# Column halves for the w_out product, column quarters for the second expert product, the combine and the stores, and fewer unused products in the drain

## The chip, the cores and the metric

The kernel runs on one core of a Trainium2 chip. The metric is the device time of one execution in microseconds (us), median of three runs. TensorE (PE), VectorE (DVE), ScalarE (ACT) and the DMA queues work side by side and are tied by semaphores. All data are fp32.

## The reference, cut to what matters

Three layers follow each other. First a chunked attention with eight memory keys (4 batches, 8 heads, 768 positions, 64 wide). Then a dense layer with a rational activation, then a soft mixture of 8 experts with 4 slots each:

```python
# x: 3072 x 512, the attention's output
h = x @ w_in                                   # 3072 x 2048
g = (a0 + a1*h + a2*h*h + a3*h*h*h) / (1 + abs(b0)*abs(h) + abs(b1)*h*h + 1e-6)
y = g @ w_out                                  # 3072 x 512
logits = y @ phi                               # 3072 x 32
d = softmax(logits, axis=0)                    # over all tokens
slot_input = (d.T @ y).reshape(8, 4, 512)
for e in range(8):
    slot_out[e] = maximum(slot_input[e] @ w1[e], 0) @ w2[e]      # 512 -> 1024 -> 512
c = softmax(logits, axis=1)                    # over the 32 slots
out = c @ slot_out                             # 3072 x 512
```

The softmax over all tokens means that no expert can start before the last token is through. w1 and w2 hold 16.8 MB each, and the output 6.3 MB.

## The kernel before, in words

**The stream of tiles.** The 3072 tokens are 24 tiles of 128 (`N`). For each tile TensorE makes the attention's scores and products, transposes, the hidden layer in four parts of 512 columns (`hidden`, lines 413 to 429, three products for each block: w_hi and w_lo, x_hi and x_lo), transposes of g (`g_transposes`, L355 by its helper), the logits by the folded weights w_out phi (`logits`, L449), and `slots` (L472), the running sum of d.T g. `step` (lines 492 to 564) interleaves the work of tiles n to n + 2. x_hi and x_lo each have two places, for even and odd tiles.

**The drain.** After the last tile, `step(B, 0)` and `step(B, 1)` finish what is left of tiles 22 and 23. Between the products that wait for other engines stand unused ones on constants (`spin_drain`, L361), four, three and one in a place.

**The slot stage.** The accumulator is transposed, copied (L888), multiplied by w_out over all 512 columns (L599, 16 products, four blocks f of four), scaled and copied to `sip` (L893), turned by four products (L605) and copied to `siT` (L895).

**The experts.** Expert weights stream through a ring of 11 stages (lines 106 to 130) of 2 MB, each of two pairs of halves; a half is 0.5 MB. Places are cut from memory that earlier phases leave: w_hi and w_lo, the attention's inputs, x, hs, g and wout. All loads and stores are issued by SyncE (lines 258 to 346), in order, each behind a wait for what frees its place. Stages 0 to 7 hold w1, 8 to 15 w2. `expert_hidden` (L615) makes the hidden slots of two groups of four experts, one expert in each 32-column strip of TensorE's array (128*32); `expert_turns` transposes them.

**Second product, combine, stores.** `expert_out` (L652) multiplies by w2. Its stages are ordered by column half `ch` of the 512 output columns, group and half of the hidden rows: stages 8 to 11 give columns 0 to 255, 12 to 15 the rest, in products 256 columns wide. VectorE adds the two groups under masks (L1140, L1143), `slot_rows` (L661) spreads the 32 rows, ScalarE copies them to `s_rows` (L912), and `combine` (L681) multiplies by the transposed c: a 32-row strip for each of four token tiles (32*128). A copy out of PSUM takes one bank, two token tiles of 256 columns. VectorE and ScalarE take turns (L1148, L916), 12 copies for each half, over banks that come round after 5 or 7. There are nine stores: three of 1 MB for the first half, six of 0.5 MB for the second. The order on TensorE is written out at lines 686 to 709:

```python
            expert_out(13, (0, 1))
            slot_rows(0)
            expert_out(13, (2, 3))
            combine(0, 0)
            expert_out(14)
            combine(0, 1)
            expert_out(15, (0, 1))
            combine(0, 2)
            expert_out(15, (2, 3))
            slot_rows(1)
            for a in range(PAIRS // 4):
                combine(1, a)
```

Of the kernel before, what the change touches and what calls it, by code (L numbers as in the profile page):

```python
# [5 lines left out]
def build(nc, qT_d, kw_d, vw_d, w_in, w_out, w_outT, cst_d, w1, w2, out):  # L6
    f32 = mybir.dt.float32
# [10 lines left out]
    N = B * T  # L18
# [11 lines left out]
    with ExitStack() as ctx:  # L30
# [23 lines left out]
        x_hi = sb("x_hi", [P, 2, KD * P], f32r)  # L54
        x_lo = sb("x_lo", [P, 2, KD * P], f32r)
# [18 lines left out]

        xn = sc
# [28 lines left out]
        assert offset["x_hi"] >= in_att + ATT * QB and offset["hs"] >= in_att + (ATT + LATE) * QB  # L104
# [5 lines left out]
        pairs += [in_att + QB * ATT, in_g, in_tmp, in_wout, in_wout + 2 * QB, (in_tmp + 2 * QB, in_wout + 7 * QB)]  # L110
# [17 lines left out]
        def landings(stage):  # L128
# [3 lines left out]
        HC = DM // 2  # L132
        PAIRS = N // 2
        o_place = [nc.alloc_sbuf_tensor_at("o_a", [P, 8, 2 * HC], f32, offset=in_wout),
                   nc.alloc_sbuf_tensor_at("o_b", [P, 4, 2 * HC], f32, offset=in_tmp + QB),
                   nc.alloc_sbuf_tensor_at("o_c", [P, 12, 2 * HC], f32, offset=in_early)]

        def o_out(ch, j):
            if ch:
                return o_place[2][:, j, :]  # L140
            return o_place[0][:, j, :] if j < 8 else o_place[1][:, j - 8, :]
# [14 lines left out]
        o_bank = [at[:, 0, :], at[:, 1, :], gb[:, :], at[:, 2, :], sl[:, :], hb[:, 0, :], hb[:, 1, :]]  # L156
        o_banks = (5, 7)
        h_banks = [hb[:, 0:2, :], at[:, 0:2, :]]
        y_bank = [[at[:, 2, :], sl[:, :]], [hb[:, 0, :], hb[:, 1, :]]]
# [94 lines left out]

        block = ctx.enter_context(nc.Block())
# [3 lines left out]
        def _(sp):  # L259
            def load_pair(stage, x, part=None):  # L260

                i = stage - 8
                src = w1[2 * (stage // 4) + x, stage % 4] if i < 0 else w2[i // 4, 2 * (i // 2 % 2) + x, i % 2]
# [33 lines left out]
            for n in range(2, N):  # L297
                load_qk(n)
                load_v(n)
                if n < 2 + EARLY // 2:  # L300
                    load_pair((n - 2) // 2, n % 2)
                elif n == 2 + EARLY // 2:
                    sp.dma_start(place(3, 0), w1[0, 3][:, 0:QUARTER]).then_inc(stage_ready[3], 16)
# [7 lines left out]
            sp.dma_start(place(3, 1), w1[0, 3][:, QUARTER:2 * QUARTER]).then_inc(stage_ready[3], 16)  # L311
# [7 lines left out]
            load_pair(8, 0)  # L319
# [4 lines left out]
            sp.wait_ge(si_psum, 1)  # L324
            load_pair(9, 1)
            sp.wait_ge(si_psum, 2)
            load_pair(10, 0)
            sp.wait_ge(si_psum, 4)
# [10 lines left out]
            STORES = ((0, 0, 4), (0, 4, 4), (0, 8, 4)) + tuple((1, 2 * k, 2) for k in range(6))  # L339
            for ch, j, count in STORES:  # L340
                sp.wait_ge(o_dve, PAIRS // 2 * ch + (j + count) // 2)
                sp.wait_ge(o_act, PAIRS // 2 * ch + (j + count) // 2)
                where = o_place[2] if ch else o_place[j // 8]
                k = j if ch else j % 8
                sp.dma_start(out[ch, :, j:j + count, :], where[:, k:k + count, :]).then_inc(stored, 16)
            sp.wait_ge(stored, 16 * len(STORES))
# [3 lines left out]
        def _(pe):  # L350
# [116 lines left out]
            def slots(b, t):  # L467
                n = b * T + t
                pe.wait_ge(dk_sb, n + 1)
                need(pe, acc_done, n)  # L470
                for f in range(FC):
                    i = mm(sl[NS * f:NS * f + NS, :], dk[:, :], g[:, t % 3, 512 * f:512 * f + 512],  # L472
# [19 lines left out]
            def step(b, t):  # L492
# [104 lines left out]
            for f in range(FC):  # L597
                for j in range(4):
                    i = mm(sl[NS * j:NS * j + NS, :], aT[:, j, NS * f:NS * f + NS], wout[:, 4 * f + j, :],  # L599
                           start=f == 0, stop=f == FC - 1)  # L600
                i.then_inc(si_psum, 1)
            spin_drain(B, 2, 3)
            pe.wait_ge(si_sb, 1)
            for kd in range(KD):
                i = mm(mb[:, NS * kd:NS * kd + NS], sip[:, kd * P:kd * P + P], srep[:, 0:NS], start=True, stop=True)  # L605
            i.then_inc(siT_psum, 1)
            spin_drain(B, 2, 1)
# [32 lines left out]
            def expert_out(stage, js=range(4)):  # L640
                ch, grp, fth = (stage - 8) // 4, (stage - 8) // 2 % 2, stage % 2
                cs = slice(HC * ch, HC * ch + HC)
                if js[0] == 0:
                    pe.wait_ge(stage_ready[stage], 32 if stage == 15 else 16 * landings(stage))
                for j in js:
                    ft = 4 * fth + j
                    if ch == 0 and j == 0:
                        pe.wait_ge((hT_act, hT_dve)[fth], grp + 1)
                    if stage == 15 and j == 2:
                        pe.wait_ge(last_ready, 32)  # L650
                    for c in range(4):
                        i = mm(y_bank[ch][grp][NS * c:NS * c + NS, 0:HC], hT[grp][:, ft, NS * c:NS * c + NS],  # L652
                               place(stage, c // 2 * 2 + j // 2)[:, HC * (2 * (c % 2) + j % 2):][:, 0:HC], start=ft == 0, stop=ft == FET - 1)
                if js[-1] == 3:
                    i.then_inc(stage_used, 1)

            def slot_rows(ch):
                cs = slice(HC * ch, HC * ch + HC)
                pe.wait_ge(y_sb, 2 * ch + 2)
                pe.wait_ge(hT_dve, 2)  # L660
                mm(mb[:, cs], srep[:, :], so[:, cs], start=True, stop=True).then_inc(rep_psum, 1)  # L661

            def combine(ch, a):
                cs = slice(HC * ch, HC * ch + HC)
                if a == 0:
                    pe.wait_ge(s_kept, ch + 1)
                if ch == 0 and a == 0:
# [3 lines left out]
                nb = o_banks[ch]  # L671
                for m in range(2):
                    for r in range(4):
                        j = 4 * a + r
                        q = PAIRS * ch + (j - nb if j >= nb else -1)
                        if m == 0 and q >= 0:
                            pe.wait_ge((o_dve, o_act)[q % 2], q // 2 + 1)
                        if m == 0 and q >= 1:
                            pe.wait_ge((o_act, o_dve)[q % 2], (q + 1) // 2)
                        rows = slice(NS * r, NS * r + NS)  # L680
                        i = mm(o_bank[j % nb][:, HC * m:HC * m + HC], cT[rows, 2 * a + m, :], s_rows[rows, cs],  # L681
# [524 lines left out]
```

## Time and profile before

| | us |
|---|---|
| median of three runs | 519.40 (519.39 to 519.45) |
| the profiled execution | 519.27 |
| its span on the core | 517.5 |
| TensorE busy | 503.0 |
| VectorE busy | 441.0 |
| ScalarE busy | 399.0 |

The span is what the profile covers; the profiled execution's own time is 1.8 us longer. In the page's second part the span is cut into 40 slices of 12.9 us, and a digit gives the busy share in tenths. A matmul of fp32 data stands as two records, and a row's `x` counts records. In a row of the timeline, the first number is the start in us, the second is the time from the first start to the last end, and `[0.34 <-DVE dk L994]` says that the engine had been idle and for what. `128*32` is the strip of the array that a product uses.

### The profile page before, as it was taken

What the parts mean: (1) busy time and instruction counts of PE and PEld (TensorE: products, weight loads), DVE (VectorE), ACT (ScalarE), POOL (GpSimd) and SP (SyncE); (2) the same over time, 40 slices, a digit from 0 to 9 for tenths busy, and PEclk for the clock granted to TensorE, in tenths of its full rate; (3) what the DMA queues carried; (4) which work ended last, traced back from release to release, by engine and by line L of the source; (5) the groups of instructions that cost most, each with busy time, mean ns of one, the idle gap of its engine ahead of it and who ended that gap; (6) DMA issues with size and microseconds to landing.
All of it is one profiled execution on the core that took longest, in us unless ns stands there. A gap on an engine that the chain in (4) does not pass through costs nothing.

```text
span 517.5 us, 15763 instructions
## 1 busy us (share of the span) xinstructions
PE 503.0 (97%) x6568; PEld 380.1 (73%) x6568; DVE 441.0 (85%) x821; ACT 399.0 (77%) x776; POOL 0.2 (0%) x4
## 2 busy tenths in 40 slices
PE   8899999999999999999999999999999999999993
PEld 7667777877787787778778777877877787654552
DVE  4898999999999999999999999999999999951133
ACT  2877989888888988888898888889888988921122
POOL 0000000000000000000000000000000000000000
PEclk9999999999999999999999999999999999999997
DMA  8982275366313122311313232131322214999998
GB/s 343 418 355 98 90 267 196 95 243 229 119 64 105 42 91 75 97 51 63 104 44 93 72 80 68 63 104 44 100 66 72 75 43 141 424 420 408 417 365 348
DMA packets 18934, 85.29 MB, mean 165 GB/s; under 512 B 2096, under 2 KB 2224, under 8 KB 13488
## 3 DMA queue, kind: packets, MB, share of 16 engines
q1 hardware_dynamic: 18720, 84.09, 44.2%
q8 instruction: 52, 0.85, 0.7%
q10 hardware_dynamic: 144, 0.20, 0.1%
q14 instruction: 18, 0.15, 0.1%
HBM read 77.99 MB, written 6.29 MB: 163 GB/s over the span
## 4 chain that ended last, share of the span: by engine, by line
PE 92%; ACT 2%; DMA 2%; DVE 1%; issue 1%; SPq 0%; DVEq 0%; ACTq 0%
PE hb L425 17%; PE hb L427 17%; PE hb L426 17%; PE gb L355 10%; PE sl L472 4%; PE at L355 4%; PE mb L449 4%; PE at L402 4%; PE at L378 3%; DMA g<-w_in 2%; PE at L615 1%; PE hb L615 1%; PE hb L652 1%; PE mb L457 1%; PE mb L355 1%; PE hb L361 1%
## 5 line engine op out<-in xcount | busy, mean ns | idle before, releaser
L425 PE MATMUL hb<-w_hi,x_hi 128*128 128x512 f32 x384 | 160.2, 417 | 0.8 <-DVE x_lo L955 0.8
L427 PE MATMUL hb<-w_hi,x_lo 128*128 128x512 f32 x384 | 151.7, 395 | 0.0
L426 PE MATMUL hb<-w_lo,x_hi 128*128 128x512 f32 x384 | 151.4, 394 | 0.0
L742 ACT ACTIVATE hs<-hb 128x512 f32<-128x512 f32 x96 | 57.2, 596 | 44.3 <-PE hb L427 44.3
L427 PEld LDWEIGHTS hb<-w_hi,x_lo 128*128 128x128 f32 x384 | 72.1, 188 | 17.7
L425 PEld LDWEIGHTS hb<-w_hi,x_hi 128*128 128x128 f32 x384 | 72.2, 188 | 15.0 <-issue 2.0
L426 PEld LDWEIGHTS hb<-w_lo,x_hi 128*128 128x128 f32 x384 | 72.4, 189 | 12.9
L964 DVE SCALAR_TENSOR_TENSOR h<-h,few,ab 128x512 f32<-128x512 f32 x96 | 71.9, 749 | 10.2 <-ACT h L746 9.9
L751 ACT ACTIVATE h<-h,few 128x512 f32<-128x512 f32 x96 | 70.1, 730 | 9.1 <-DVE h L964 9.1
L969 DVE SCALAR_TENSOR_TENSOR tt<-tt,cst,hs 128x512 f32<-128x512 f32 x96 | 72.2, 752 | 3.4
L979 DVE SCALAR_TENSOR_TENSOR g<-tt,cst,h 128x512 f32<-128x512 f32 x96 | 71.4, 746 | 2.3 <-ACT h L755 0.2
L744 ACT ACTIVATE ab<-hb,cst 128x512 f32<-128x512 f32 x96 | 65.8, 686 | 0.6 <-DVE h L964 0.6
L967 DVE TENSOR_TENSOR tt<-tt,hs 128x512 f32<-128x512 f32 x96 | 65.8, 685 | 0.0
L755 ACT ACTIVATE h<-h 128x512 f32<-128x512 f32 x96 | 60.7, 632 | 3.1
L355 PE MATMUL gb<-cst,g 128*128 128x128 f32 x380 | 59.7, 280 | 0.4 <-ACT gT L761 0.4
L746 ACT ACTIVATE h<-hb 128x512 f32<-128x512 f32 x96 | 57.9, 603 | 0.0
L761 ACT ACTIVATE gT<-gb 128x512 f32<-128x512 f32 x93 | 56.2, 604 | 0.7 <-PE gb L355 0.7
L962 DVE TENSOR_SCALAR tt<-hs,cst 128x512 f32<-128x512 f32 x96 | 52.1, 543 | 2.9 <-ACT hs L742 0.4
L355 PEld LDWEIGHTS gb<-cst,g 128*128 128x128 f32 x380 | 42.7, 140 | 10.4 <-issue 2.2
L355 PE MATMUL at<-cst,sc 128*128 128x128 f32 x192 | 29.7, 277 | 1.5 <-ACT sc L721 1.1
L449 PEld LDWEIGHTS mb<-gT,Wp 128*32 128x32 f32 x736 | 20.9, 110 | 13.5 <-issue 13.5
L355 PEld LDWEIGHTS at<-cst,sc 128*128 128x128 f32 x192 | 23.7, 150 | 6.1 <-ACT sc L721 1.8
(154 smaller groups left out, 540.4 us busy)
## 6 DMA issues: line engine op xcount, KB each, us to landing
place<-w SPq DMA_DIRECT2D x27, 1024.0 KB, 9.6
v_in<-v_windows SPq DMA_DIRECT2D x24, 520.0 KB, 3.7
kw<-k_windows SPq DMA_DIRECT2D x24, 512.0 KB, 4.6
qT<-q_t SPq DMA_DIRECT2D x24, 256.0 KB, 2.8
place<-w SPq DMA_DIRECT2D x10, 512.0 KB, 16.6
wout<-w_out_t SPq DMA_DIRECT2D x4, 1024.0 KB, 14.6
wout<-w_out SPq DMA_DIRECT2D x4, 1024.0 KB, 9.0
g<-w_in SPq DMA_DIRECT2D x3, 1024.0 KB, 10.3
```

The source lines that it names most:

```text
L355: return mm(dst, src, ident[0:rows, 0:rows], start=True, stop=True, is_transpose=True)
L425: mm(o, x_hi[:, p, xs], w_hi[:, f, kd, :], start=kd == 0, stop=False)
L426: mm(o, x_hi[:, p, xs], w_lo[:, f, kd, :], start=False, stop=False)
L427: i = mm(o, x_lo[:, p, xs], w_hi[:, f, kd, :], start=False, stop=kd == KD - 1)
L744: A(ab[:, :], hb[:, e, :], ACT.Abs, scale=bc[:, 0:1])
L746: A(h2[:, e, :], hb[:, e, :], ACT.Square).then_inc(h_read, 1)
L751: A(h2[:, e, :], h2[:, e, :], ACT.Ln, bias=cq[:, 0:1]).then_inc(ln_done, 1)
L755: A(h2[:, e, :], h2[:, e, :], ACT.Exp, scale=-1.0).then_inc(r_done, 1)
L964: V.scalar_tensor_tensor(out=h2[:, e, :], in0=h2[:, e, :], scalar=bm[:, 1:2], in1=ab[:, :], op0=ALU.mult, op1=ALU.add).then_inc(q_done, 1)
L967: V.tensor_tensor(tt[:, e, :], tt[:, e, :], hs[:, e, :], ALU.mult).then_inc(poly_step, 1)
L969: V.scalar_tensor_tensor(out=tt[:, e, :], in0=tt[:, e, :], scalar=pc[:, 1:2], in1=hs[:, e, :], op0=ALU.add, op1=ALU.mult).then_inc(poly_st ...
L979: V.scalar_tensor_tensor(out=g[:, t % 3, 512 * f:512 * f + 512], in0=tt[:, e, :], scalar=pc[:, 0:1], in1=h2[:, e, :], op0=ALU.add, op1=ALU ...
```

## The change: what it does

1. **x.** x_hi and x_lo become one tensor in which a tile's two halves lie together, so the place of even tiles is one half of the ring. The first half of stage 8 is issued as soon as tile 22's hidden parts are done, ahead of stages 4 to 7. The other half of that pair keeps its place behind stage 7.
2. **The drain.** Unused products 4 -> 1 and 3 -> 2 before and after the last transposes of g. The slots product of the last tile writes another PSUM bank and doesn't wait for the accumulation before it; the accumulation of tile 22 moves behind VectorE's copy of dk for tile 23.
3. **The slot stage.** The w_out product runs over columns 0 to 255, then 256 to 511, into two banks. The turn of the first half stands inside the second half, the turn of the second half behind the first stage of the expert's hidden product, and the unused products of this stage (3 and 1) go. The loads that follow si_psum wait for its new counts.
4. **Second product.** w2 is laid out on the host by column quarters (128 columns): a stage holds all 1024 hidden rows of one quarter and one group. Order of (quarter, group): (0,0) (1,0) (0,1) (1,1) (2,0) (2,1) (3,0) (3,1). A stage is 32 products of 128 columns, not 16 of 256. Both groups of a quarter share one PSUM bank.
5. **Combine, copies, stores.** For each quarter there is a set of 16 products filling four banks (four token tiles each) and one of 8 filling half of four banks. Banks come round after 5. A store follows each set: 1 MB and 0.5 MB, eight in all. The host's rearranging of the output follows.

```diff
+            def load_half(stage, half):
+                sp.dma_start(place(stage, half), (w1[half // 2, stage] if stage < 4 else w2_of(stage, half // 2))
+                             [:, QUARTER * (half % 2):QUARTER * (half % 2) + QUARTER]).then_inc(stage_ready[stage], 16)
...
+            sp.wait_ge(h_psum, (N - 1) * FC)
+            load_half(8, 0)
             for f in range(FC):
...
-            load_pair(8, 0)
+            load_half(8, 1)
...
-            sp.wait_ge(si_psum, 1)
+            sp.wait_ge(si_psum, 2)
             load_pair(9, 1)
...
+            for quarter in range(4):
+                for part in range(2):
+                    cs = slice(16 * HC * part, 16 * HC + 8 * HC * part)
+                    sp.wait_ge(o_dve, 4 * quarter + 2 * part + 2)
+                    sp.wait_ge(o_act, 4 * quarter + 2 * part + 2)
+                    sp.dma_start(out[quarter, :, cs], o_place[quarter][:, cs]).then_inc(stored, 16)
...
                 if drain:
-                    spin_drain(b, t, 4)
+                    spin_drain(b, t, 1)
                     g_transposes(*prev, 3)
-                    spin_drain(b, t, 3)
+                    spin_drain(b, t, 2)
                     logits(*prev)
...
+            def slot_turns(half):
+                pe.wait_ge(si_sb, half + 1)
+                for kd in (2 * half, 2 * half + 1):
+                    i = mm(mb[:, NS * kd:NS * kd + NS], sip[:, kd * P:kd * P + P], srep[:, 0:NS], start=True, stop=True)
+                i.then_inc(siT_psum, 1)
+            for half in range(2):
+                cs = slice(DM // 2 * half, DM // 2 * half + DM // 2)
+                for f in range(FC):
+                    for j in range(4):
+                        i = mm((sl, gb)[half][NS * j:NS * j + NS, cs], aT[:, j, NS * f:NS * f + NS], wout[:, 4 * f + j, cs],
+                               start=f == 0, stop=f == FC - 1)
+                    if half or f == FC - 1:
+                        i.then_inc(si_psum, 1)
+                    if half and f == 1:
+                        slot_turns(0)
...
+                    for j in range(4):
+                        ft = 4 * half + j
+                        for c in range(4):
+                            u = mm(y_bank[quarter % 2][NS * c:NS * c + NS, HC * grp:HC * grp + HC], hT[grp][:, ft, NS * c:NS * c + NS],
+                                   place(stage, c // 2 * 2 + half)[:, HC * (4 * (c % 2) + j):HC * (4 * (c % 2) + j) + HC],
+                                   start=ft == 0, stop=ft == FET - 1)
...
+                k = 0
+                for a in SETS[part]:
+                    for m in range(2):
+                        for r in range(4):
+                            u = o_use(quarter, part, r) - len(o_banks)
+                            if k == 0 and u >= 0:
+                                pe.wait_ge((o_dve, o_act)[u % 2], u // 2 + 1)
...
+                            i = mm(o_bank(quarter, part, r)[:, HC * k:HC * k + HC], cT[rows, 2 * a + m, :], s_rows[rows, cs],
+                                   start=True, stop=True)
...
+            expert_out(3, (0,))
+            slot_rows(0)
+            expert_out(3, (1,))
+            combine(0, 0)
+            slot_rows(1)
+            expert_out(4, (0,))
+            combine(0, 1)
+            expert_out(4, (1,))
+            combine(1, 0)
+            expert_out(5, (0,))
+            combine(1, 1)
+            expert_out(5, (1,))
+            expert_out(6, (0,))
+            slot_rows(2)
+            expert_out(6, (1,))
+            combine(2, 0)
+            expert_out(7, (0,))
+            combine(2, 1)
+            expert_out(7, (1,))
+            slot_rows(3)
+            combine(3, 0)
+            combine(3, 1)
...
+                if n == N + 1:
+                    accumulate(*tile(-3))
+                if prev2 and n not in (N - 1, N):
                     accumulate(*prev2)
...
+            def slot_sum(quarter):
+                cs = slice(HC * quarter, HC * quarter + HC)
+                dve.wait_ge(stage_used, 9 + W2_STAGES.index((quarter, 1)))
+                V.tensor_scalar(so[:, cs], y_bank[quarter % 2][:, 0:HC], emask[:, 0:1], None, ALU.mult).then_inc(y_sb, 1)
...
```

## Rows read from the trace of the kernel before

**Rows 1.** The page, second part: clock and DMA in 40 slices.
```profile
PEclk9999999999999999999999999999999999999997
DMA  8982275366313122311313232131322214999998
```

**Rows 2.** The chain of waits, from 503: start us, us, what.
```profile
503.87 0.40 DVE g L1140
...
506.08 0.55 PE at L681 x2
...
507.24 0.70 DVE o_c L1148
...
510.92 0.60 DVEq L30
```

**Rows 3.** Windows: PE, PEld, DVE, ACT, POOL busy, PEclk, DMA share, GB/s.
```profile
434.00:438.00 4.00, 4.00 (x19) 3.21 (x18) 3.64 (x7) 3.57 (x8) 0.00 (x0) 1.00 0.15 25
498.00:499.00 1.00, 1.00 (x24) 0.57 (x20) 0.84 (x2) 0.68 (x2) 0.00 (x0) 1.00 0.50 201
504.00:505.00 1.00, 0.09 (x1) 0.09 (x1) 0.75 (x2) 0.00 (x0) 0.00 (x0) 1.00 1.03 418
514.00:517.50 3.50, 0.00 (x0) 0.00 (x0) 0.00 (x0) 0.00 (x0) 0.00 (x0) 0.50 0.75 298
```

**Rows 4.** The timeline of the drain, all engines.
```profile
451.09 1.41 DVE L979 SCALAR_TENSOR_TENSOR g<-tt,cst,h 128x512 f32<-128x512 f32 x2
451.61 1.57 ACT L761 ACTIVATE gT<-at 128x512 f32<-128x512 f32 x3
...
452.38 1.06 PE L361 MATMUL hb<-cst 128*128 128x128 f32 x8
...
453.28 0.60 PE L355 MATMUL gb<-cst,g 128*128 128x128 f32 x4
...
458.06 0.33 PE L355 MATMUL hb<-cst 128*128 128x128 f32 x1
...
458.71 0.18 DVE L994 COPY dk<-hb 128x32 f32<-128x32 f32 x1
...
458.95 1.07 PE L472 MATMUL sl<-g,dk 128*32 128x512 f32 x8 [0.34 <-DVE dk L994]
```

**Rows 5.** The timeline of the slot stage, TensorE.
```profile
462.23 3.64 PE L599 MATMUL sl<-wout,gT 128*32 128x512 f32 x32
...
466.68 1.08 PE L605 MATMUL mb<-cst,g 128*128 128x32 f32 x8
...
468.12 7.07 PE L615 MATMUL hb<-place,g 128*32 128x512 f32 x64
```

**Rows 6.** The timeline of the second product and the combine, TensorE.
```profile
483.99 1.91 PE L652 MATMUL at<-place,g 128*32 128x256 f32 x32
...
492.06 2.77 PE L652 MATMUL hb<-place,g 128*32 128x256 f32 x48
494.76 0.70 PE L661 MATMUL mb<-g,cst 128*128 128x256 f32 x2
495.39 1.07 PE L652 MATMUL hb<-place,g 128*32 128x256 f32 x16
496.39 0.48 PE L681 MATMUL at<-s_rows,cT 32*128 32x256 f32 x2
...
497.46 1.93 PE L652 MATMUL hb<-place,gT 128*32 128x256 f32 x32
```

**Rows 7.** The chain of waits, one tile's logits.
```profile
432.19 0.88 PE mb L449 x32
```

**Rows 8.** Groups by form, 440 to 512 us, weight loads of the combine.
```profile
L681 PEld LDWEIGHTS at<-s_rows,cT 32*128 32x128 f32 x56 | 4.6, 183 | 2.5 <-ACT s_rows L912 0.9 <-DVE o_c L1148 0.6 <-ACT o_a L916 0.4
```

**Rows 9.** The timeline of SyncE's queue: issues.
```profile
463.36 0.33 SPq L266 DMA_DIRECT2D place<-w  x1
...
507.99 5.41 SPq L345 DMA_DIRECT2D out_dram<-o_c x6
```

More of the change, by code:

```diff
@@ L337, in _ @@
                     load_pair(15, x, part_of)
[L339 to L346, printed above, removed]
+            for quarter in range(4):
[4 more added lines that the diff above has]
+                    sp.dma_start(out[quarter, :, cs], o_place[quarter][:, cs]).then_inc(stored, 16)
+            sp.wait_ge(stored, 16 * 8)
         @block.tensor
@@ L469, in slots @@
                 pe.wait_ge(dk_sb, n + 1)
-                need(pe, acc_done, n)
+                if not (isinstance(n, int) and n == N - 1):
+                    need(pe, acc_done, n)
                 for f in range(FC):
-                    i = mm(sl[NS * f:NS * f + NS, :], dk[:, :], g[:, t % 3, 512 * f:512 * f + 512],
+                    i = mm(s_bank(n)[NS * f:NS * f + NS, :], dk[:, :], g[:, t % 3, 512 * f:512 * f + 512],
                            start=True, stop=True)
@@ L638, in combine_turns @@
                 i.then_inc(cT_psum, 1)
[L640 to L649, printed above, removed]
-                        pe.wait_ge(last_ready, 32)
[L651 to L660, printed above, removed]
-                mm(mb[:, cs], srep[:, :], so[:, cs], start=True, stop=True).then_inc(rep_psum, 1)
[L663 to L667, printed above, removed]
+            def expert_out(i, halves=(0, 1)):
+                quarter, grp = W2_STAGES[i]
+                stage = 8 + i
+                for half in halves:
+                    if half == 0:
+                        pe.wait_ge(stage_ready[stage], 32 if stage == 15 else 16 * landings(stage))
+                    elif stage == 15:
+                        pe.wait_ge(last_ready, 32)
+                    if quarter == 0:
+                        pe.wait_ge((hT_act, hT_dve)[half], grp + 1)
+                    for j in range(4):
[4 more added lines that the diff above has]
+                                   start=ft == 0, stop=ft == FET - 1)
+                if half == 1:
+                    u.then_inc(stage_used, 1)
@@ new lines, in slot_rows, with combine @@
+            def slot_rows(quarter):
+                cs = slice(HC * quarter, HC * quarter + HC)
+                pe.wait_ge(y_sb, 2 * quarter + 2)
+                if quarter == 0:
+                    pe.wait_ge(hT_dve, 2)
+                    pe.wait_ge(cT_dve, 1)
+                mm(mb[:, cs], srep[:, :], so[:, cs], start=True, stop=True).then_inc(rep_psum, 1)
+            def combine(quarter, part):
+                cs = slice(HC * quarter, HC * quarter + HC)
+                if part == 0:
+                    pe.wait_ge(s_kept, quarter + 1)
+                if quarter == 0 and part == 0:
@@ L670, in combine @@
                     pe.wait_ge(cT_dve, 1)
[L671 to L681, printed above, removed]
-                               start=True, stop=True)
-                        if m == 1:
-                            i.then_inc(o_psums, 1)
-            for kd in range(KD):
-                expert_hidden(0, kd)
+                k = 0
[5 more added lines that the diff above has]
+                                pe.wait_ge((o_dve, o_act)[u % 2], u // 2 + 1)
+                            rows = slice(NS * r, NS * r + NS)
+                            i = mm(o_bank(quarter, part, r)[:, HC * k:HC * k + HC], cT[rows, 2 * a + m, :], s_rows[rows, cs],
+                                   start=True, stop=True)
+                            if k == 2 * len(SETS[part]) - 1:
+                                i.then_inc(o_psums, 1)
+                        k += 1
+            expert_hidden(0, 0)
+            slot_turns(1)
+            expert_hidden(0, 1)
+            pe.wait_ge(siT_sb, 2)
+            expert_hidden(0, 2)
+            expert_hidden(0, 3)
             expert_hidden(1, 0)
```

157 lines of the change are left out of this document (82 added, 75 removed).

## The prediction
> **What bounds the kernel now.** I read the page first, then the busy time by stretches, then the chain of waits of the end, then the instructions in order of time. On the page the reader is to see TensorE busy in nearly every slice at the full granted clock, and the DMA line going to 9 over the last sixth [rows 1]. So there are two candidates behind about 440 us. In the chain of waits the loads do not appear: TensorE works through the second expert product with its data landed, and the last load is done when the DMA share falls to one half at 498 to 499 us [rows 3], while the last product ends at 503.87 us. What follows is a serial tail [rows 2]: slot rows on VectorE, a spread product, a copy on ScalarE, the combine from 506.08, the first copy out of PSUM at 507.24, the first of six stores at 507.99 [rows 9], the last copy at 510.92, and then only data moving: 3.15 MB left to store after 507.99. The share of 0.75 over the last 3.5 us, next to about 1.03 at full load [rows 3], puts the last byte at 514 + 3.5 x 0.75/1.03 = 516.6 us, 0.9 before the end of the span. At the 418 GB/s of a full stretch [rows 3] 3.15 MB take 7.5 us, so the data began 1.1 us behind the first issue. The tail from the last product to the end is 13.6 us, of which 7.5 is half of the output going out in one stretch. It is the tail's stores and TensorE's path to them that count; the steady state up to 450 us is not touched.
>
> **The drain (450 to 461 us).** Four unused products go. Each is two records, 0.11 us a record: 8 records stand from 452.38 to 453.28 [rows 4], so 0.22 to 0.225 each. The fourth part's transposes stood behind four of them. Their input, g of the last part, is ready at 451.09 + 1.41 = 452.50 [rows 4]; with one product they start at 452.60 and not at 453.28: 0.68 us. ScalarE's copy of them and the logits follow at the same distance, since ScalarE is done with the three earlier copies by about 453.2. The other product removed lay in that copy's shadow. Second, VectorE's copy of dk for the last tile at 458.71 stood behind an accumulation, while its transpose had ended at 458.39; the slots product started at 458.95 after 0.34 us of idling [rows 4]. Now the copy goes first, the product writes another bank and waits for no accumulation, and it starts 0.3 us sooner. The accumulation moved behind it, about 0.7 us like the 512-column copy [rows 2], lies beside a slots product of 1.07 and is hidden; if it weren't, at most 0.7 returns. Together 1.0 us. Bounds: 0.3 (the copies are the gate after all) and 1.0, and I take 1.0, because the rows name each gate.
>
> **The w_out product in halves (462 to 468 us).** Before, the product starts at 462.23, then come three unused products, the turn of sip (8 records from 466.68), one more unused product, and the first expert product at 468.12 [rows 5]: 5.89 us. The halves stream the same columns: 64 records of 256 columns take 3.46 us in another place (48 of them 492.06 to 494.76) [rows 6], as 32 of 512 do here, so 3.64 stays. ScalarE's copy of the first half (0.52 for 512 columns [rows 4]) lies beside 0.91 us of the second half's products. What is left on the path is half of the turn, 4 records, 0.52 us, and two changes of the array's shape. I price those from the same rows: 16 records of the second product take 1.00 us where 16 x 0.0541 = 0.87 would do [rows 6], so 0.13 a change. 3.64 + 0.52 + 0.26 = 4.4 us: 1.5 gained. The second half of the turn comes back behind the first hidden stage at 0.52 + 0.26 = 0.8. Net 0.7. TensorE then comes to the second expert product 1.7 us sooner, 482.3 instead of 483.99.
>
> **Loads.** Half of one stage is now asked for when tile 22 has left its x place, into a stretch where DMA is 0.15 busy [rows 3]: 0.5 MB, 1.25 us, off the saturated stretch. One load that waited for the first quarter of the w_out product is issued at about 463.6 instead of 463.36 [rows 9], since a row block is only free after its second half; the queue has work until about 464.3 by then, and data follow an issue by about a microsecond, so at most 0.5 us of the gain is lost. Before, the last load was done at about 498.5; now it is at 497 to 497.5. Its user comes behind 502, so loads stay hidden; what they cost if TensorE gained 5 us more is another matter.
>
> **The second product, combine and stores by quarters.** Product: 512 records of 128 columns. The form exists: 32 records of the logits take 0.88 us [rows 7], 0.0275 each, so 14.1 us in all, where 256 columns gave 0.0541 x 256 = 13.9. Combine: before, 16 records from 496.39 to 497.46 [rows 6], 1.07 us, of which 0.85 is streaming (0.0535 a record, as in the product) and 0.2 the change. With 128 columns no row shows it. Lower bound: 0.0275 a record, half the streaming, the logits' own interval. Upper bound: 0.0535, nothing saved, because the loaded weights stay 128 columns wide at 0.18 us a load [rows 8] and are twice as many. I take 0.0275: the load overlaps between the four row groups already (four loads of 0.183 pass in 4 x 0.0535 = 0.21), and 128-wide loads with 128 columns pass at 0.11 in the unused products [rows 4]; four groups side by side make 0.0275. Slot rows: the before form took 0.63 (494.76 to 495.39) [rows 6] for 256 columns; with half 0.42, and there are three before the last product's end instead of one.
>
> Path from the start of the second product to its end, after: products 14.1, nine pieces followed by another shape x 0.13 = 1.2, the turn of the hidden part 1.0 as before, slot rows 3 x 0.42 = 1.3, combine 144 records x 0.0275 = 4.0 and 6 x 0.2 = 1.2, and two waits of 0.25 where a combine's second set needs the bank whose copy is VectorE's second (two copies of 0.65 against a 1.0 us half stage). Sum 23.2 us; before it was 503.87 - 483.99 = 19.9. The last product ends at 482.3 + 23.2 = 505.5, which is 1.6 us later than now.
>
> **Tail after.** From the last product to the combine now 2.21 us [rows 2]; with 128 columns each of the four steps shortens, estimated 1.7. Combine of the first set: 32 records 0.9 and 0.3 of latency; two VectorE copies 0.7 + 0.6; store issued at 505.5 + 1.7 + 1.15 + 1.3 = 509.7. The second set waits for those copies, 0.5 and 0.8 us, issued at 511.0, while the first set's data still move. Data: 509.7 + 1.1, then 1.57 MB in 3.8 us: 514.6. With 0.9 the span ends at 515.5. Earlier quarters don't hold it up: 497.3 + 4.7 MB in 11.4 us is 508.7, before 510.8. The span shortens by 2.0 to 2.1 us; the profiled execution took 519.27, 1.77 of it around the span of 517.5, so 517.2. The median of the runs, 519.40, is 0.13 above the profiled one, less than I can resolve.
>
> **Rivals.** (1) *The combine becomes bound by weight loads.* Each combine product keeps 128 stationary columns, and there are 96 instead of 48. If 0.0535 a record stands, 144 x 0.026 = 3.7 us are added before the last product's end and 0.8 + 0.2 behind it: 517.2 + 4.7 = 521.9, slower. It decides from about 0.039 a record, where the gain is gone. For: the load row is 0.183 us, longer than half the streaming. Against: four pass in 0.21 already. The Trainium skill, page "TensorE: Matmul & The Clock Gate", section "Part 2: What happens when you issue a matmul", says that loading weights costs by the number of columns and not by rows, so a 32-row load costs as much as a full one; by its 107 ns per 128 columns and with nothing in parallel the combine alone would take 192 x 0.107 = 20.5 us, an estimate from that page. The trace disagrees with the serial form, since 16 records take 1.07 with everything [rows 6], where that form would need 1.7. Chance 0.12.
> (2) *The removed unused products hid real waits*: TensorE then idles where it spun, the 0.7 us of the drain and 0.3 of the w_out stage don't come: 518.2. For: ScalarE's three copies (to 453.18) end close to the new start. Chance 0.15.
> (3) *Changes of shape overlap with following loads*, or the eviction waits vanish: 1 to 1.5 us less, 515.9. The limit is the data: 497 + 15.1 for all stores + 0.9 = 513, or 514.8 as a time. Chance 0.12.
> (4) *The clock.* It was granted at the full 2.4 GHz throughout, through the idle 0.9 us at 504 too [rows 3], and stands at one half (1.2 GHz) only in the last stretch, with no product left [rows 3]. With eight unused products fewer, a fall in the drain would double some 4 us of work: 521. Chance 0.03.
> (5) *The diff does nothing*: the tail is moved, not shortened, 519.2. Chance 0.05.
>
> **Numbers.** Forecast 0.53 for 517.2, own range 516.4 to 518.2. 0.2% is 1.04 us and about what can be told from no change, so faster means under 518.4: forecast, (3) and most of (2): 0.77. Same: a piece of (2) and (5), 0.08. Slower: (1), (4): 0.15. Range 515.4 to 519.4: it takes in (2), (3) and (5), and leaves out (1) and (4).
>
> **What would show it.** The transposes of the last part at 452.6 (not 453.3); the first expert product at about 465.6 and the second at 482.3; the combine's 16 records in 0.65 us, 32 in 1.1 (at 0.0535: 1.05 and 1.9); the last product's end at 505.5; stores of the last quarter issued at 509.7 and 511.0; a DMA pause before 510.8. The prediction is wrong if the last product ends beyond 507.5, if loads stop TensorE in stages 14 or 15, or if DMA is busy without pause from 440 us to the end, in which case data and not TensorE set the end.

## The result and the profile after

The changed kernel takes 522.33 us (521.92 to 522.70), the kernel before 519.39 (519.30 to 519.45) beside it: a ratio of 1.0055 (1.0043 to 1.0067). It is slower by 2.9 us where 2.2 us less were forecast. The profiled execution took 522.7 us, its span 520.9.

The page, second and third part:
```profile
PE   8899999999999999999999999999999999899884
PEclk9999999999999999999999999999999999999999
DMA  8992275367223122312322131322223117999996
q8 instruction: 55, 0.90, 0.7%
```
TensorE's line of the kernel before:
```profile
PE   8899999999999999999999999999999999999993
```
Against [rows 1] the DMA line has the same shape, and the clock is full in the last slice too. TensorE's line has 8s where the kernel before had 9s: in the slice of the drain (442.8 to 455.8 us), whose unused products are gone, and in the two from 481.8 to 507.9, where the second product and the combine are. The page doesn't say why. Queue 8 carries instructions: 55 packets of 16 KB, 52 in the kernel before.

The chain of waits says it (start us, us, what):
```profile
490.81 2.06 issue
...
497.92 1.33 issue
...
503.94 0.95 issue
...
511.21 0.36 DVE g L1201
...
512.00 0.50 PE mb L691 x2
...
512.86 0.37 PE hb L709
...
514.06 1.28 DVE o L1210 x2
...
516.35 0.33 DVEq L30
```
The lower part answers to [rows 2]: sum, spread, combine and copies, in the forecast's order and close to its length. The upper three lines are new. "issue" is time in which the engine waited for nothing that the profile shows. The timeline of TensorE shows where they lie:
```profile
452.70 0.60 PE L375 MATMUL gb<-cst,g 128*128 128x128 f32 x4
...
458.09 1.06 PE L493 MATMUL at<-g,dk 128*32 128x512 f32 x8
...
461.37 1.93 PE L628 MATMUL sl<-wout,gT 128*32 128x256 f32 x32
...
464.10 0.63 PE L621 MATMUL mb<-cst,g 128*128 128x32 f32 x4
...
482.08 1.93 PE L679 MATMUL at<-place,g 128*32 128x128 f32 x64
...
489.53 0.49 PE L691 MATMUL mb<-g,cst 128*128 128x128 f32 x2
489.94 0.86 PE L679 MATMUL sl<-place,gT 128*32 128x128 f32 x24
492.87 0.42 PE L679 MATMUL sl<-place,gT 128*32 128x128 f32 x8 [2.06 <-issue]
493.23 0.38 PE L709 MATMUL at<-s_rows,cT 32*128 32x128 f32 x2
...
494.33 0.49 PE L691 MATMUL mb<-g,cst 128*128 128x128 f32 x2
...
497.43 0.49 PE L709 MATMUL hb<-s_rows,cT 32*128 32x128 f32 x4
499.25 0.38 PE L709 MATMUL at<-s_rows,cT 32*128 32x128 f32 x2 [1.33 <-issue]
...
503.12 0.83 PE L679 MATMUL sl<-place,g 128*32 128x128 f32 x20
504.90 0.63 PE L679 MATMUL sl<-place,g 128*32 128x128 f32 x12 [0.95 <-issue]
```
The first rows answer to [rows 4 and 5], the others to [rows 6]. TensorE stops 24 records into a run of 32, 4 records into a combine set, and 20 records into another run. In the two runs the program has no wait between one product and the next. In the combine set it has one, for the copy out of the next bank, and it was met before the stop at 497.92; this is the last copy, done at 497.25:
```profile
496.84 0.41 DVE L1210 COPY o<-at 128x256 f32<-128x256 f32 x1
```
So no wait of the kernel's is the reason. And each time the stop costs more than its idle time: the 32 records around the first take from 489.94 to 493.23, 3.29 us, where an undisturbed run takes 1.01; the 32 combine records around the second 2.91 where the set from 493.23 to 494.33 took 1.10; the 32 around the third 2.34 instead of 1.01. Together 2.28 + 1.81 + 1.33 = 5.4 us.

Taken off, 511.18 - 5.4 = 505.8 is left for the last product's end (forecast 505.5) and 522.7 - 5.4 = 517.3 for the execution (517.2). That is arithmetic and not a run: E4 and E5 below lose the stops and take 517.90 and 518.20. The first question is what the three stops are.

Windows of TensorE between the stops (columns as in [rows 3], x counts records):
```profile
482.00:490.80 8.80, 8.80 (x262) 7.71 (x254) 2.09 (x4) 1.47 (x3) 0.00 (x0) 1.00 1.02 414
...
492.87:497.90 5.03, 5.03 (x126) 3.90 (x127) 2.75 (x6) 1.91 (x5) 0.00 (x0) 1.00 1.01 403
499.25:503.90 4.65, 4.65 (x128) 3.98 (x128) 2.54 (x6) 1.75 (x4) 0.00 (x0) 1.00 0.99 405
...
505.00:510.00 5.00, 5.00 (x126) 3.98 (x125) 1.33 (x3) 1.36 (x3) 0.00 (x0) 1.00 0.33 134
```
From one stop to the next TensorE runs 126 + 127 = 253 and 128 + 128 = 256 records of products and weight loads; its few semaphore instructions are not in these counts. And just ahead of each restart one packet of the instruction queue passes. The DMA view of 490 to 491 (packets, MB, share of 16 engines):
```profile
q1 hardware_dynamic: 102, 0.41, 100.8%
q8 instruction: 1, 0.02, 6.9%
```
6.9% of 16 engines for 1 us is one engine for 1.1 us. Its packets stand from 490.50, 496.73 and 502.43, each about 1.1 us long, and TensorE goes on 1.26, 1.41 and 1.44 us after their end. From 483 to 502 the blocks are some 7, 6.2 and 5.7 us apart, at 99 to 103% of data traffic; once the loads are done (505 to 510, share 0.33) they come at 506.5 and 510.5, 4 us apart, and TensorE doesn't stop.

That gave theory F: TensorE runs out of instructions. The second product in 128 columns has 1.7 times as many instructions per microsecond (262 + 254 in 8.8 us, 59 a us, against 35 before), a block of some 256 lasts 4.4 to 5 us, and among full data queues a block comes every 5.7 to 6.2. The kernel before, in one window of the same phase:
```profile
485.00:494.00 9.00, 9.00 (x161) 5.43 (x152) 1.66 (x3) 0.60 (x1) 0.00 (x0) 1.00 1.01 414
```
Same DMA share, 35 records a us: a block lasts 7.4 us. The Trainium skill, page "Runtime: NRT & Kernel Launch", section "Instruction fetch mechanics", says that instructions come in 16 KiB blocks of 256, fetched by the sequencer's own DMA queue; the 253 and 256 records agree. It also calls the cost of a block's border "mostly hidden", since the sequencer hands out instructions slower than they are fetched. By that the three stops would be nothing; the trace shows 5.4 us.

### The profile page after: what moved, and what is told of

It reads as the page before. It is cut to its first block, busy times and chain, and to the rows that moved or that the text cites. A ratio compares the mean times of both kernels' runs of the same rounds, so it can differ in the third digit from the quotient of the medians.

```text
span 520.9 us, 16502 instructions
## 1 busy us (share of the span) xinstructions
PE 504.2 (97%) x6940; PEld 387.3 (74%) x6940; DVE 442.3 (85%) x829; ACT 400.1 (77%) x784; POOL 0.2 (0%) x4
## 4 chain that ended last, share of the span: by engine, by line
PE 92%; ACT 2%; DMA 2%; issue 1%; DVE 1%; SPq 0%; DVEq 0%; ACTq 0%
PE hb L445 17%; PE hb L447 17%; PE hb L446 17%; PE gb L375 10%; PE at L375 4%; PE sl L493 4%; PE mb L469 4%; PE at L422 3%; PE at L398 3%; DMA g<-w_in 2%; PE sl L679 2%; PE at L679 1%; PE at L641 1%; PE hb L641 1%; PE mb L477 1%
## 5 line engine op out<-in xcount | busy, mean ns | idle before, releaser
L445 PE MATMUL hb<-w_hi,x 128*128 128x512 f32 x384 | 160.0, 417 | 0.9 <-DVE x L1014 0.9
L447 PE MATMUL hb<-w_hi,x 128*128 128x512 f32 x384 | 151.5, 394 | 0.0
L446 PE MATMUL hb<-w_lo,x 128*128 128x512 f32 x384 | 151.4, 394 | 0.0
L447 PEld LDWEIGHTS hb<-w_hi,x 128*128 128x128 f32 x384 | 71.9, 187 | 17.7
L445 PEld LDWEIGHTS hb<-w_hi,x 128*128 128x128 f32 x384 | 72.2, 188 | 15.5 <-issue 2.3
L446 PEld LDWEIGHTS hb<-w_lo,x 128*128 128x128 f32 x384 | 72.4, 188 | 13.1
L375 PEld LDWEIGHTS at<-cst,sc 128*128 128x128 f32 x192 | 23.7, 150 | 6.0 <-ACT sc L764 1.6
```

The costliest lines, as they stand in the source:

```text
L375: return mm(dst, src, ident[0:rows, 0:rows], start=True, stop=True, is_transpose=True)
L445: mm(o, x_hi[:, p, xs], w_hi[:, f, kd, :], start=kd == 0, stop=False)
L446: mm(o, x_hi[:, p, xs], w_lo[:, f, kd, :], start=False, stop=False)
L447: i = mm(o, x_lo[:, p, xs], w_hi[:, f, kd, :], start=False, stop=kd == KD - 1)
```

## Experiments

Ratios are to the kernel before on the same chip (519.51 us beside E1 to E4, 519.32 beside E5 to E9). In the texts on record F is the fetch theory and the other letters are the rivals described there.

| | us | ratio | stops, us |
|---|---|---|---|
| E1: x place, drain, slot stage only | 518.14 | 0.9974 (0.9965 to 0.9983) | none |
| E2: quarters only | 522.87 | 1.0066 (1.0052 to 1.0080) | 1.61, 1.18 |
| E3: before, stages 8 to 11 in twice the instructions | 521.73 | 1.0042 (1.0026 to 1.0057) | 2.40 |
| E4: after, late loads at one eighth | 517.90 | 0.9968 (0.9956 to 0.9980) | none |
| E5: first half as before, last half in quarters | 518.20 | 0.9978 (0.9969 to 0.9987) | none above 0.3 |
| E6: after, two loads under way | 529.68 | 1.0197 (1.0166 to 1.0228) | 1.28 |
| E7: E5, two loads under way | 525.46 | 1.0124 (1.0109 to 1.0140) | none |
| E8: E1, two loads under way | 528.58 | 1.0169 (1.0138 to 1.0199) | none |
| E9: after, early stores at one eighth | 521.43 | 1.0042 (1.0025 to 1.0059) | 1.83, 1.33 |

**E1. Parts 1 to 3 of the change alone.** The second product, combine and stores stay as before.
```diff
-                    spin_drain(b, t, 4)
+                    spin_drain(b, t, 1)
...
+            load_half8(0)
...
+            for half in range(2):
+                cs = slice(DM // 2 * half, DM // 2 * half + DM // 2)
...
+                    if half and f == 1:
+                        slot_turns(0)
```


> The kernel before with the x place, the drain and the slot stage of the change; second product, combine and stores as before. Theory F (TensorE runs out of instructions in the second product: the loss is in three idle stretches marked issue, 5.4 us in all, where half-width products double its instructions while the DMA engines are full of data): none of those stretches here, the second product starts at 482.1, and the whole tail moves by the 1.7 to 1.9 us gained: 517.5 us. Rival D (the loads, or the stores behind them, hold up whatever TensorE gains): TensorE comes sooner but the end stays within 0.5 us of before, 519.0.

Measured 518.14, faster by 1.4 us. TensorE's timeline of E1:
```profile
482.28 1.91 PE L667 MATMUL at<-place,g 128*32 128x256 f32 x32
...
493.05 0.70 PE L676 MATMUL mb<-g,cst 128*128 128x256 f32 x2
...
496.22 1.93 PE L667 MATMUL hb<-place,gT 128*32 128x256 f32 x32 [0.40 <-DMA place<-w]
```
The second product begins 1.71 us earlier than in [rows 6], the 1.7 that was forecast. The median gained 1.4 of it: 0.4 is lost to stage 14's load, which in the kernel before landed in time. So these parts work, and in this order of stages a load is no longer hidden after about 1.3 us of gain.

**E2. Parts 4 and 5 alone**: the change with parts 1 to 3 set back to what the kernel before has.
```diff
-                    spin_drain(b, t, 1)
+                    spin_drain(b, t, 4)
...
-            sp.wait_ge(h_psum, (N - 1) * FC)
-            load_half(8, 0)
```


> The changed kernel with drain, slot stage and the early half load put back as before; quarters kept. Theory F: the three idle stretches come again (4 to 6 us), nothing gained ahead of them, so about 1.8 us above the changed kernel, 524.1 us. Rival D: what was gained ahead of the second product was lost to loads anyway, so the time is that of the changed kernel, 522.3.

Measured 522.87: the quarters by themselves are slower by 3.4 us. E2's chain of waits:
```profile
493.58 1.61 issue
495.19 0.37 PE hb L702
...
500.20 1.18 issue
501.37 0.49 PE at L702 x4
```
Two stops and not three, which is most of why it lies 1.2 below what was expected. Between them 127 + 128 = 255 records run (495.19 to 500.20): a block again. Instruction packets stand at 492.71 and 498.87, and TensorE goes on 1.46 and 1.42 us after their ends. The first stop falls 16 records of products later in the program than in the change (8 records into a combine set, not 24 into the run ahead of it). The program ahead of it is shorter by as many: the w_out product has 32 records where the change has 64, and the unused products put 16 back. Counted from the program's start it is the same place (see below).

**E3. The density alone.** The kernel before, but its stages 8 to 11 are multiplied as two products of 128 columns each. The arithmetic, the combine and all stores stay.
```diff
-                    for c in range(4):
...
+                    for part in range(1 if ch else 2):
+                        w = HC if ch else P
+                        for c in range(4):
+                            i = mm((y_bank[ch][grp], hb[:, grp, :])[part][NS * c:NS * c + NS, 0:w], hT[grp][:, ft, NS * c:NS * c + NS],
+                                   place(stage, c // 2 * 2 + j // 2)[:, HC * (2 * (c % 2) + j % 2) + w * part:][:, 0:w],
+                                   start=ft == 0, stop=ft == FET - 1)
...
+            pe.wait_ge(y_sb, 2)
+            expert_out(12)
```


> The kernel before with one edit: in the first column half (stages 8 to 11) each product of 256 columns is made as two of 128, into two banks, so 128 products where 64 were, with the same columns streamed; VectorE adds the halves with four instructions instead of two. Order, loads and stores as before. Theory F: from 484 to 491.5 the stream is as dense in instructions as in the changed kernel and the DMA engines as full, so an idle stretch marked issue of 1 to 2.5 us appears between 488 and 495, and the time is 521 us. Rival Q (the quarter order itself, its waits on banks, rows and stages, is what costs): no such stretch, at most 0.3 us for the changes: 519.7.

Measured 521.73, 2.2 us slower. The stretch ahead of the stop, and the timeline of TensorE:
```profile
485.00:492.20 7.20, 7.20 (x237) 6.83 (x233) 1.30 (x3) 0.60 (x1) 0.00 (x0) 1.00 1.02 415
...
492.18 0.81 PE L654 MATMUL hb<-place,g 128*32 128x256 f32 x9
495.39 2.36 PE L654 MATMUL hb<-place,g 128*32 128x256 f32 x39 [2.40 <-issue]
```
The stretch has 65 records a us, and behind it comes one stop of 2.40 us, against a loss of 2.2. The added wait for y_sb isn't it: the stop comes 9 records behind it, inside stage 12. It comes behind the dense stretch, in products 256 columns wide that the kernel before ran without one: a product's form is not the reason, the number of instructions before it is. An instruction packet stands from 492.81 to 493.89, and TensorE goes on 1.50 us later. This is the cleanest run of the study.

**E4. The traffic alone.** The changed kernel, every instruction kept, but loads of stages 11 to 15 move one eighth of their bytes.
```diff
+                if stage >= STAGES:
+                    cut = QUARTER // 8
...
+                        sp.dma_start(place(stage, 2 * x + half)[:, 0:cut], src[:, QUARTER * half:QUARTER * half + cut]
```


> The changed kernel, but of stages 11 to 15 only an eighth of each load's columns is moved (8.75 MB of loads are left out, so the output lacks their data); instructions on TensorE are the same. Theory F with contention (instruction blocks come late because the DMA engines are full of data): DMA is nearly idle from about 478 until the stores, the idle stretches at 490.8 and 497.9 go, and with them 4 us or more: 516 to 518 us. Rival N (the stream is too dense for instruction fetch whatever else moves): both stretches stay, 522 us. Rival L (TensorE waits for late loads): the stretches go too, but then they must stand ahead of a stage's first product, while in the changed kernel the first stands 24 records into a half stage.

Measured 517.90, 4.4 us under the change. Windows of E4:
```profile
485.00:490.00 5.00, 5.00 (x164) 4.60 (x162) 1.39 (x3) 0.39 (x1) 0.00 (x0) 1.00 0.02 5
490.00:495.00 5.00, 5.00 (x142) 4.13 (x144) 2.60 (x6) 2.10 (x6) 0.00 (x0) 1.00 0.14 56
495.00:500.00 5.00, 5.00 (x152) 4.25 (x146) 2.54 (x6) 1.84 (x5) 0.00 (x0) 1.00 0.95 382
```
TensorE is busy without a gap at up to 65 records a us, so density alone doesn't stop it. In the third row the stores fill the DMA engines (0.95) and it still goes on: one block came late there (packets at 491.1, then 497.6), and more than one block's worth was used between them. So a block is in store behind the one at work. It was just enough: the late packet ended at 498.43, and TensorE came to its first instruction at 499.86, 1.43 us later, as close as at a stop.

**E5. A hybrid.** Columns 0 to 255 as before, 256 to 511 as two quarters; parts 1 to 3 kept.
```diff
-        W2_STAGES = ((0, 0), (1, 0), (0, 1), (1, 1), (2, 0), (2, 1), (3, 0), (3, 1))
+        UNITS = (slice(0, 256), slice(256, 384), slice(384, 512))
...
+                if i < 4:
+                    grp, fth = i // 2, i % 2
...
+                            u = mm(y_bank[0][NS * c:NS * c + NS, 256 * grp:256 * grp + 256], hT[grp][:, ft, NS * c:NS * c + NS],
```


> x place, drain and slot stage as in the change; the first 256 output columns as before (stages 8 to 11 in products of 256 columns, one combine of three sets, 3 MB of stores), the last 256 as two quarters with the change's last stages, order and stores. TensorE has 192 products of the second kind where before has 128 and the change 256. Theory F: no idle stretch marked issue up to 489; after that the stream is dense and the DMA engines are full until 498, so one stretch, 1.5 to 2.5 us; the last product's end at 504.5 to 506.5 and a tail of 9.8 us: 517.5 us, and 515.7 if no block comes late. Rival S (the gain of quarters is nothing, since stores only wait for each other): the time is not under that of the kernel with the first three parts alone, 518.1.

Measured 518.20, level with E1. The one stop that F expected didn't come. Its windows:
```profile
490.00:495.00 5.00, 4.75 (x114) 3.42 (x110) 1.44 (x3) 0.81 (x2) 0.00 (x0) 1.00 1.02 415
495.00:500.00 5.00, 5.00 (x116) 3.61 (x108) 3.71 (x8) 2.60 (x6) 0.00 (x0) 1.00 1.02 408
500.00:505.00 5.00, 5.00 (x132) 4.09 (x132) 2.15 (x5) 2.02 (x6) 0.00 (x0) 1.00 1.03 424
505.00:510.00 5.00, 3.11 (x72) 2.26 (x62) 2.28 (x5) 1.60 (x4) 0.00 (x0) 1.00 1.00 416
```
At 45 records a us and a share of 1.02 block and supply meet (256 records in 5.7 us), and 53 a us pass for the 5 us from 500. The stops are gone, the last product ends at 505.8, and yet E1 isn't beaten: the DMA share is 0.99 to 1.03 in every 5 us from 465 to 510, the case that the forecast's last sentence names. From the last product's end to the span's end E5 takes 10.5 us where the change, with its share of 0.33 from 505 to 510, takes 9.7: 0.8 us that the traffic costs. That data alone set the end at about 518 is likely by this share, but no run lightens the stores of E5 or E1; the forecast's rival 3 put that limit at 514.8.

**E6, E7, E8. Fewer loads under way.** If full queues delay the block, loads held back to two at a time should let it through. From stage 11 on, each load waits until the one two places before it has landed; done to the change (E6), the hybrid (E7) and E1 (E8).
```diff
                 for x in range(2):
+                    sp.wait_ge(pair_ready[stage - 1, x, 0], pair_count(stage - 1, x))
                     load_pair(stage, x)
```


> The changed kernel, but from stage 11 on a 1 MB load is issued only when the one before the last has landed, so at most two are under way instead of four to eight; the bytes and TensorE's instructions are the same. Theory F, queue depth (an instruction block waits behind the data already queued): the first two idle stretches shrink to under 1 us together, 519 us. Theory F, share (the block is late whenever the DMA engines are full, however little is queued): the stretches stay, 522.3 us.

> The hybrid of two column widths with the loads held to two under way. Queue depth: its idle stretch shrinks, 516.0 us. Share: as the hybrid, within 0.3 us.

> The kernel with the first three parts alone, where TensorE waited 0.4 us for stage 14, with the loads held to two under way. If loads that are under way together share the engines and so land together and late, stage 14 lands 2 us sooner and the wait goes: 517.6 us. If they land in the order of issue, holding them back gains nothing or leaves gaps in the DMA share: 518.1 us or more.

All three missed, and by far: 529.68, 525.46 and 528.58. Only the second case for E8, "518.1 us or more", holds, and it didn't foresee 10 us. E6's waits of TensorE (total, times, longest):
```profile
PE sl L691 <- DMA place<-w: 2.7, 1, 2.7
PE hb L721 <- issue: 1.3, 1, 1.3
```
and E8's:
```profile
PE hb L681 <- DMA place<-w: 4.1, 2, 2.8
```
With two under way the loads ran at 323 to 372 GB/s between 480 and 498 instead of 415, and TensorE waited for them. A second cost came with it, in E6's windows:
```profile
505.00:510.00 5.00, 2.29 (x55) 1.66 (x56) 2.04 (x4) 1.81 (x4) 0.00 (x0) 0.96 0.87 298
510.00:515.00 5.00, 3.78 (x54) 3.04 (x58) 0.70 (x2) 0.28 (x1) 0.00 (x0) 0.50 1.03 428
```
TensorE was busy for 2.29 of 5 us, and then its granted clock is one half (1.2 GHz): 54 records in 3.78 us. In E8, too, the granted clock is 0.58 from 498 to 500, behind a wait of 2.8 us. The times of these kernels scatter by 4 to 7 us (E6 526.99 to 531.92, E7 524.84 to 530.69, E8 524.27 to 531.36), and the traces of E6 and E8 are from their fastest executions, that of E7 from its slowest, so the medians are not explained to a microsecond. Of the fetch theory they say little. In E6 the stops shrink from 4.35 to 1.28 us, the way queue depth forecast it, but the DMA share was lower as well (0.93 and 0.97 in the 5 us on either side of 490), so depth and share aren't told apart. No figure of F rests on these runs; holding the loads to two under way is refuted as a remedy.

**E9. Which traffic?** The changed kernel, stores of the first three quarters moving one eighth.
```diff
+                    if quarter < 3:
+                        cs = slice(cs.start, cs.start + (cs.stop - cs.start) // 8)
```


> The changed kernel, but of the stores of quarters 0 to 2 only an eighth of the columns is moved (4.1 MB of the output are left out); loads and TensorE's instructions are the same. Theory F with contention: the two idle stretches that fall while loads fill the DMA engines (490.8 and 497.9) stay, the third (503.9, beside stores alone) goes with its 1.4 us of the path: 521.0 us. If it is the density alone (rival N) all three stay: 522.3. If the blocks come late only because of loads, the third stays too.

Measured 521.43, 0.9 under the change. Its timeline of TensorE:
```profile
492.93 0.43 PE L681 MATMUL sl<-place,gT 128*32 128x128 f32 x8 [1.83 <-issue]
...
499.31 0.38 PE L711 MATMUL at<-s_rows,cT 32*128 32x128 f32 x2 [1.33 <-issue]
```
The first two stops stay, at the same instructions; the third, around which DMA is now 0.20 busy (500 to 505), is gone. The last product ends at 509.94, 1.2 us sooner. With E4 this puts the first two down to the loads and the third to the stores; the last load had landed at 500.6 in the change.

**All stops by the count of instructions.** This is counted in the traces, over all records of TensorE: products, weight loads and semaphore instructions. The stops of the change stand behind record 13249, 13505 and 13761, those of E2 behind 13249 and 13505, that of E3 behind 13249, that of E6 behind 13505, those of E9 behind 13249 and 13505. That is nine stops in five kernels, at quite different instructions, each at 193 plus a multiple of 256. And each of the eleven kernels has as many packets on queue 8 as it has such borders: 52 before, 53 in E3, 55 in the change. No wait of the program follows such a count; a block's end does.

Paired with the borders in order, so that a stop's packet is the one just ahead of its restart, the packets show two more things in all eleven traces. TensorE never passes a border sooner than 1.26 us after the end of its packet. And the packet for the next border never starts more than 2.4 us before TensorE passes this one, so there is at most one block in store behind the one at work. With that the first stop can be added up: TensorE passes the border before it at 486.52, the next packet starts 3.98 us later, lasts 1.11, and 1.26 go by until the restart, 6.35 in all; the block at work lasted 4.29 (to 490.81), and 2.06 of idling are left. The times from a border to the next packet's start were 3.98, 3.86 and 3.18 us ahead of the change's stops and 3.87 ahead of E3's, but 0.34 and 0.44 in E4 at DMA shares of 0.02 and 0.14. In the kernel before they were 1.09 and 1.95 at a share of 1.01, beside blocks of 7.4 us and more. In E2 the third packet came 2.06 us behind its border (share 0.86) and ended 1.82 before it was needed: there is no third stop.

E1 and E5 beat both kernels; between them nothing can be told (0.9974 and 0.9978, the intervals overlap). E1 is the simpler.

## Why the prediction was wrong

It said 517.2, the kernel took 522.33. By the forecast's own steps:

- **The drain**: transposes at 452.70 (forecast 452.60), the last slots product at 458.09, 0.86 before [rows 4] where 1.0 was taken. Right. Rival 2, that the removed products hid waits, is wrong: the start didn't slip.
- **The w_out product in halves**: it started at 461.37, the first expert product at 465.55, the second product at 482.08 (forecast 465.6 and 482.3). Right, and E1 shows the 1.7 us alone.
- **Loads**: no load stopped TensorE in the changed kernel, as forecast, nor in E5, which has the same last stages and no stops; E1, in the old order of stages, pays 0.40 us. But the time of the last load was misread from a DMA share of one half: it landed at 500.44 in the kernel before, not at 498.5, and at 500.58 in the change, not at 497 to 497.5.
- **The combine**: 32 records in 1.10 us, 16 in 0.65 (496.41 after 495.76). Right, and rival 1 (1.9 and 1.05) is wrong, though its 521.9 is closest to the result. A time that fits isn't a cause that fits.
- **The tail**: from the last product's end, 511.18, to the span's end 9.7 us; forecast 10.0. Right for a kernel that was held up before it. "Earlier quarters don't hold it up" fails where nothing was held up: the forecast pause in the traffic is there in the change (share 0.33 from 505 to 510) and not in E5 (1.00), whose tail is 10.5.
- **"Products 14.1", and the combine's 4.0 us of streaming: this is the step that failed.** It took 512 and 144 records at the interval of the logits' 32 [rows 7], a burst of 0.88 us in a stretch where DMA is 0.15 busy [rows 3], and made a stream of 14 us out of it beside a share of 1.02. The interval held, 64 records take 1.75 us; the supply did not. The sum had no term for instructions themselves. Missing: 5.4 us, shown by the stops in the trace, by E3 (more instructions only: a stop of 2.40 and 2.2 us lost) and by E4 (less traffic only: no stop). No rival named it. The forecast's first sign of being wrong, a last product's end beyond 507.5, came true at 511.18.

The stops are not quite all of it. E4 gets back 4.4 of the 5.1 us between 522.33 and 517.2, E5, which moves all bytes but has another first half, 4.1. In E4 the way from the second product's start (482.24) to its end (506.16) is 23.9 us where the sum has 23.2; in E5 the tail is 0.5 longer than forecast.

The balance: parts 1 to 3 gain 1.4 (E1). The quarters shorten the tail by 3.9 us (13.6 before, 9.7 after) and lengthen the way from the second product's start to its end from 19.9 to 23.7 (482.08 to 511.18, less 5.4), so without stops they would gain about 0.1, an estimate that E5 against E1 bears out; the forecast's own terms gave them 0.3. With their stops they lose 3.4 (E2).

Open: when a block is requested, which the trace doesn't show, so whether the 3 to 4 us go by in the queue or before it.

## What to carry to other kernels

Count instructions per microsecond where DMA is full, and not only bytes and columns. Here 35 to 45 records a us of TensorE's products and weight loads passed beside a DMA share of about 1.02, and 53 for 5 us; 59 over 8.8 us (the change) and 65 over 7.2 us (E3) did not. Halving a product's width doubles that number at no change in streaming time. When a profile shows "issue" in the middle of a run of like products, look for instruction packets just ahead of the restart before looking for a semaphore. A count of all TensorE records at two such stops settles it: here they are 256 apart. And when a change gains time on the engine that is ahead of full DMA queues, ask what the queues can still give: E5 ends its last product where the change would have without stops, and still only matches E1.

## What the runs showed of the hardware that was not expected

- TensorE's instruction blocks move beside the data: from its passing a border to the next packet's start it took 0.34 and 0.44 us at DMA shares of 0.02 and 0.14 (E4), and 3.2 to 4.0 us ahead of the stops, at about 1.0. A packet lasts 1.1 us.
- Nine stops in five kernels all stand at 193 plus a multiple of 256 instructions of TensorE. No border was passed sooner than 1.26 us after its packet's end, and never was more than one block in store behind the one at work.
- Two loads of up to 1 MB under way gave 323 to 372 GB/s (E6 and E8), the unthrottled queue 415: an idea meant to give a 16 KB packet room cost 7 us (E6 against the change, by medians).
- TensorE's clock stayed full through stops of 2.06 and 2.40 us, and was granted at one half (1.2 GHz) behind the wait of 2.69 us in E6.
- Combine products of 32 rows, each record with a weight load of 185 ns, pass at 1.10 us for 32 records in four row groups: the loads, 5.9 us in sum, lie side by side.
